# An attention scan and two feed-forward blocks on one core: another order for the first units, and levels in pairs

## The reference, cut to what matters

```
# q, k, v, f_logit: (4, 8, 768, 48), float32
f = sigmoid(f_logit)
for t in range(768):
    state = f[t][:, None] * state + outer(k[t], v[t])     # per batch and head, 48 x 48
    y[t] = q[t] @ state
x = y as (3072, 384)
h = x @ w_in                                              # 384 -> 2048
g = h if h >= 1, 0 if h <= -1, else (h + 1)**2 / 4
x = g @ w_out                                             # 2048 -> 384
out = (silu(x @ w_gate) * (x @ w_val)) @ w2_out           # 384 -> 1536 -> 384
```

## Time and profile before

| | |
|---|---|
| time, median of 3 runs | 1065.81 us (1065.61 to 1066.0) |
| the profiled execution's own time | 1066.25 us |
| its span, first to last instruction | 1064.0 us |
| TensorE busy | 1001.3 us, 94% |
| VectorE, ScalarE, GpSimd busy | 509.1, 457.1, 450.7 us |
| unit 0's scan alone | 0 to 75.08 us |
| stage 0 with unit 1's scan | 75.08 to 175.97 us |
| one later stage with a scan | 94.4 us |
| stage 5 and the second block | 553.80 to 1064.0 us |
| sizes of the opening loads (page, part 6) | gates, queries, keys 512 KB a group; q_tok, k_tok 384; eye 64; mask 80 |

### The profile page before, as it was taken

How to read it: one execution, slowest core, us unless ns; L and a number is a source line. 1 busy time by engine, 2 the same in 40 slices (tenths; PEclk the granted TensorE clock), 3 DMA queues, 4 the chain that set the end, 5 groups by cost and what they waited for, 6 DMA issues and landing times.

```text
span 1064.0 us, 19376 instructions
## 1 busy us (share of the span) xinstructions
PE 1001.3 (94%) x8008; PEld 818.2 (77%) x8008; DVE 509.1 (48%) x625; ACT 457.1 (43%) x832; POOL 450.7 (42%) x368
## 2 busy tenths in 40 slices
PE   2467899999999999999999999999999999999997
PEld 2455687778777777877888888888888888888886
DVE  7946955863793596478427522222222222222221
ACT  3459548556654855575436522122122222222221
POOL 4957963763665376356328312112112122122121
PEclk9979999999999999999999999999999999999999
DMA  9423005005101400410044010010010000000000
GB/s 359 161 88 132 1 14 207 31 2 178 72 2 38 182 31 2 131 59 2 15 165 149 30 60 1 1 60 1 1 60 1 26 34 1 30 1 1 30 1 30
DMA packets 17366, 63.50 MB, mean 60 GB/s; under 512 B 1920, under 2 KB 2176, under 8 KB 16512
## 3 DMA queue, kind: packets, MB, share of 16 engines
q1 hardware_dynamic: 17280, 62.28, 16.1%
HBM read 52.84 MB, written 9.44 MB: 59 GB/s over the span
## 4 chain that ended last, share of the span: by engine, by line
PE 82%; POOL 6%; issue 5%; ACT 3%; DVE 2%; DMA 1%; SPq 0%; POOLq 0%; ACTq 0%; DVEq 0%
PE acc L487 10%; PE acc L489 10%; PE acc L488 10%; PE bank L514 7%; PE bank L515 7%; PE bank L513 7%; PE hid L473 5%; PE hid L475 5%; PE hid L474 5%; PE bank L360 5%; PE hid L514 2%; PE hid L515 2%; PE hid L513 2%; POOL g_lo L989 2%; POOL keys L950 2%
## 5 line engine op out<-in xcount | busy, mean ns | idle before, releaser
L996 POOL TENSOR_TENSOR g_lo<-prod,g_hi 128x512 fp32r<-128x512 f32 x72 | 93.0, 1292 | 347.5 <-ACT g_hi L710 347.5
L989 POOL TENSOR_TENSOR g_lo<-act_tmp,g_hi 128x512 fp32r<-128x512 f32 x96 | 137.3, 1431 | 178.0 <-ACT g_hi L671 178.0
L892 DVE TENSOR_TENSOR sig<-sig,bank 128x512 f32<-128x512 f32 x72 | 49.5, 687 | 275.4 <-ACT sig L704 275.4
L710 ACT CAST g_hi<-prod 128x512 fp32r<-128x512 f32 x72 | 44.7, 621 | 247.8 <-PE acc L489 247.8
L950 POOL TENSOR_TENSOR keys<-keys,gates 128x512 f32<-128x512 f32 x82 | 110.4, 1347 | 47.5 <-PE bank L360 30.7
L810 DVE COPY_PREDICATED scores<-mask,bank 64x512 f32<-64x512 int32 x120 | 116.4, 970 | 20.3 <-PE bank L360 19.0
L671 ACT CAST g_hi<-act_tmp 128x512 fp32r<-128x512 f32 x96 | 59.5, 619 | 152.6 <-DVE act_tmp L880 152.6
L487 PE MATMUL acc<-g_hi,wout_hi 128*128 128x512 f32 x288 | 117.3, 407 | 7.4 <-POOL g_lo L989 7.4
L473 PE MATMUL hid<-x_hi,win_hi 128*128 128x512 f32 x288 | 118.4, 411 | 5.9 <-DVE act_tmp L880 5.9
L475 PE MATMUL hid<-x_hi,win_lo 128*128 128x512 f32 x288 | 113.2, 393 | 0.0
L474 PE MATMUL hid<-x_lo,win_hi 128*128 128x512 f32 x288 | 113.1, 393 | 0.0
(11 more groups left out here) (83 smaller groups left out, 1862.7 us busy)
## 6 DMA issues: line engine op xcount, KB each, us to landing
gates<-in_f_dram SPq DMA_DIRECT2D x12, 512.0 KB, 5.3
queries<-in_q_dram SPq DMA_DIRECT2D x12, 512.0 KB, 4.6
keys<-in_k_dram SPq DMA_DIRECT2D x12, 512.0 KB, 5.2
values<-in_v_tok_dram SPq DMA_DIRECT2D x6, 1024.0 KB, 8.5
q_tok<-in_q_tok_dram SPq DMA_DIRECT2D x12, 384.0 KB, 9.1
k_tok<-in_k_tok_dram SPq DMA_DIRECT2D x12, 384.0 KB, 9.6
x_dram<-x_out SPq DMA_DIRECT2D x6, 768.0 KB, 3.2
x_raw<-x_dram SPq DMA_DIRECT2D x6, 768.0 KB, 5.5
```

The lines of the kernel that those rows point to most:

```text
L989: pool.tensor_tensor(g_lo[:, c % RING, :], act_tmp[:, 2 + c % 2, :], g_hi[:, c % RING, :].bitcast(F32), ALU.subtract).then_inc(g_lo_done, 1)
```

## The change

1. **Opening loads.** For each group, gates, queries and keys now come before q_tok and k_tok; the identity and the mask come after all five of group 0.
2. **Unit 0's plan** is written out. The gates come first, then the copies of the first level; diagonals are summed and placed between the first levels; each `take_level` comes one step later behind the next scaling; GpSimd splits no weights during the levels; `key_values` and what follows lie in stage 0, behind its first `hidden`.
3. **Counting.** `q_gated` is a semaphore of its own, and unit 0 no longer does its last two scalings of queries, so its `outputs` do not wait for them. `keys_tok` of unit 0 has a place of its own.
4. **Unit 1.** Its plan has pairs from half slot 4; its diagonals are placed by VectorE, no longer by ScalarE; its gates are loaded before its keys, and both loads of gates and queries wait for earlier points.
5. **Weights' low parts.** GpSimd's pieces 0 to 3 of w_in come after unit 0's levels and 4 to 7 in chunks 0 to 3 of stage 0; the 8 pieces of w_out go to VectorE, in chunks 1 to 8. `state_apart` is cleared by GpSimd.
6. **Pairs.** In units 1 to 5 the two steps of a level are in one half slot on TensorE and for `scale_q`; copies, takes and `scale_k` keep one half slot each. All four `outputs` are in one half slot. `last` and the diagonals move by a slot.

```diff
@@ plans
-H_FIRST = -9
+H_FIRST = -13
+BY_VECTOR = 2
-USUAL = usual((1, 3, 5, 7, 8, 9, 10, 12, 13, 14), 16, 18, 21)
-SECOND = usual((6, 8, 9, 10, 11, 12, 13, 14, 16, 17), 19, 21, 23, place=(0, 2, 3, 4), sigmoid=(3, 4), gated=(4, 5))
-FIRST = USUAL._replace(diag=(-3, -2), sigmoid=(-3, -2), gated=(-3, -2))
+FIRST = Plan(own=(-6, -3), diag=(-4, 1), place=(-2, 2), sigmoid=(-6, -5), gated=(-6, -3),
+             copy=(-6, -4, -2, 0, 2, 4, 6, 8, 10, 12, 14, 14), step=(-4, -2, 0, 2, 4, 6, 8, 10, 12, 14),
+             take=(0, 2, 4, 6, 8, 10, 12, 14, 16, 18), scale=(-5, -1, 1, 3, 5, 7, 9, 11, 13, 15, 17, 17),
...
+SECOND = usual((4, 7, 10, 13, 15), 18, 21, 23, own=(-11, -10), diag=(-10, -9), place=(-8, 1), sigmoid=(-7, -6),
+               gated=(-6, -5))
+USUAL = usual((2, 5, 8, 11, 13), 16, 19, 21)
@@ usual: was place=(-6, -5, -4, -3), copy = step-1, take = step+1, y=(y, y, y+1, y+1)
+    two = [h for h in levels for _ in range(2)]
+    p = Plan(own=(-13, -12), diag=(-12, -11), place=(-7, -6, -5, -4), sigmoid=(-2, -1), gated=(-1, 0),
+             copy=[h + g - 2 for h in levels for g in range(2)] + [whole - 1] * 2, step=two,
+             take=[h + g + 1 for h in levels for g in range(2)], scale=two + [whole] * 2 + [last] * 2,
+             turn=[h + g for h in levels + (whole, last) for g in range(2)], whole=whole, whole_take=whole + 1,
+             last=last, last_take=last + 1, decay=y + 1, y=(y, y, y, y), y_out=(y, y, y + 1, y + 1),
@@ SyncE
         for g in range(2):
-            load_tok(0, (g,))
             load_f(0, (g,))
-            if g == 0:
-                sp.dma_start(eye[:, :], ident).then_inc(const_in, 16)
             load_q(0, (g,))
             load_k(0, (g,))
+            load_tok(0, (g,))
             if g == 0:
+                sp.dma_start(eye[:, :], ident).then_inc(const_in, 16)
                 sp.dma_start(mask[:, :], masks).then_inc(mask_in, 16)
@@ TensorE, outputs
                 pe.wait_ge(v_in, 16 * (a + 1))
-                pe.wait_ge(q_scaled, (a + 1) * SCALED_A_UNIT)
                 if a > 0:
+                    pe.wait_ge(q_scaled, scaled(a, SCALES))
@@ VectorE
-        dve.memset(state_apart[:, :, :].rearrange("p x d -> p (x d)"), 0.0).then_inc(cleared, 1)
...
+                if m == 0 and 1 <= c < 1 + W2N:
+                    split_w2(c - 1)
@@ GpSimd
+        pool.memset(state_apart[:, :, :].rearrange("p x d -> p (x d)"), 0.0).then_inc(cleared, 1)
...
-            if h >= 4 and h % 2 == 0 and h // 2 - 2 < W1N:
-                split_w1(h // 2 - 2)
+            if h == 19:
+                split_w1(0)
+            elif 23 <= h < 26:
+                split_w1(h - 22)
...
-                if m == 0 and c < W2N:
-                    split_w2(c)
+                if m == 0 and c + 4 < W1N:
+                    split_w1(c + 4)
```

More of the change, by code:

```diff
@@ L49 @@
 DVE_A_UNIT, ACT_A_UNIT = STEPS + 2, 3 + B
-SCALED_A_UNIT = 2 + SCALES
 HS = 32
-H_FIRST = -9
+H_FIRST = -13
+BY_VECTOR = 2
 Plan = namedtuple("Plan", "own diag place sigmoid gated copy step take scale turn whole whole_take last last_take "
                           "decay y y_out tk tk_out kv state state_place")
[L62 to L69, removed]
+FIRST = Plan(own=(-6, -3), diag=(-4, 1), place=(-2, 2), sigmoid=(-6, -5), gated=(-6, -3),
+             copy=(-6, -4, -2, 0, 2, 4, 6, 8, 10, 12, 14, 14), step=(-4, -2, 0, 2, 4, 6, 8, 10, 12, 14),
+             take=(0, 2, 4, 6, 8, 10, 12, 14, 16, 18), scale=(-5, -1, 1, 3, 5, 7, 9, 11, 13, 15, 17, 17),
+             turn=(-4, -2, 0, 2, 4, 6, 8, 10, 12, 14, 16, 16, 18, 18), whole=16, whole_take=17, last=18, last_take=19,
+             decay=20, y=(20, 20, 20, 20), y_out=(20, 20, 21, 21), tk=(22, 22, 22, 22), tk_out=(22, 22, 23, 23),
+             kv=HS, state=HS + 1, state_place=HS + 2)
@@ new lines, in usual @@
+def usual(levels, whole, last, y, **others):
+    two = [h for h in levels for _ in range(2)]
[4 more added lines that the diff above has]
+             last=last, last_take=last + 1, decay=y + 1, y=(y, y, y, y), y_out=(y, y, y + 1, y + 1),
+             tk=(y + 2, y + 2, y + 3, y + 3), tk_out=(y + 3, y + 3, y + 4, y + 4), kv=y + 4, state=y + 5, state_place=y + 6)
@@ L88, in turns @@
 def turns(m, h):
-    if m < 0:
-        return [(0, h)] + [(1, p) for p in range(H_FIRST, 0) if h == p + HS - 8]
-    now = []
+    now = [(0, h + HS)] if m == 0 else []
     if m + 1 < UNITS:
@@ L102, in fill, with scaled @@
     return a * FILLS + i
+def scaled(a, n):
+    return sum(SCALES if b else COPIES for b in range(a)) + n
 def merges(a, s):
@@ L426, in turn_keys @@
             pe.wait_ge(k_scaled, a * SCALES + SCALES - 1 + b // 2)
+            if a == 0 and b == 0:
+                pe.wait_ge(const_in, 16)
             for p in range(PAIRS):
@@ L438, in key_values @@
                     d = e * (P - D)
-                    last = pe.matmul(of(a, i)[rows(e), x * D:(x + 1) * D], keys_tok[:, bp, e, :],
+                    last = pe.matmul(of(a, i)[rows(e), x * D:(x + 1) * D], keys_tok[min(a, 1)][:, bp, e, :],
                                      values[:, bp, d:d + D], start=True, stop=True)
@@ L626, in attention @@
         def attention(a, h):
-            for b in range(B):
-                if a > 0 and PLANS[a].place[b] == h:
+            if a >= BY_VECTOR:
+                for b in placed(PLANS[a].place, h):
                     place_diag(a, b)
-            for g in range(2):
-                if PLANS[a].sigmoid[g] == h:
-                    sigmoid(a, g)
+            for g in placed(PLANS[a].sigmoid, h):
+                sigmoid(a, g)
             if h == PLANS[a].whole_take:
@@ L763, in gated @@
             t = group(queries, g)
-            dve.tensor_tensor(t, t, group(gates, g), ALU.mult).then_inc(q_scaled, 1)
+            dve.tensor_tensor(t, t, group(gates, g), ALU.mult).then_inc(q_gated, 1)
         def sum_own(a, g):
@@ L959, in attention @@
         def attention(a, h):
-            for g in range(2):
-                if PLANS[a].own[g] == h:
-                    own(a, g)
+            for g in placed(PLANS[a].own, h):
+                own(a, g)
             for s in placed(PLANS[a].turn, h):
```

62 lines of the change are left out of this document (35 added, 27 removed).

## The result

| | before | changed |
|---|---|---|
| median of 4 runs, us | 1065.9 | 1049.57 (1048.31 to 1050.42) |
| ratio, 95% interval | | 0.9842 [0.9825, 0.9859] |
| profiled execution, us (span) | 1066.25 (1064.0) | 1048.31 (1046.4) |
| first `hidden` | 75.08 | 69.17 |
| hidden chunk 10 of stage 0 | 138.70 | 136.02 |

The single steps were worse than the total: the start (units 0 and 1) gave 3.05 us of the span instead of 6.8, the later stages 14.55 instead of 4.7 (175.97 + 888.03 = 1064.0 before; 172.92 + 873.48 = 1046.4 now). One miss of 3.8 and one of 9.9 of opposite sign made the total look better than its parts; that is luck.

The account below looks back on a forecast made before the run. Gains were seen in unit 0's latency, TensorE's idle time in unit 1 (VectorE taken as full) and later stages, mostly TensorE's own work. Chunk 10 -6.6, outputs -0.2, later stages -4.7: -11.5, so 1054.3 us, range 1045 to 1061.

Parts of the forecast that it names:

- the 1.15 taken: Unit 0, VectorE: each scaling falls from 1.57 to 1.15 us with GpSimd's pieces gone, 12 x 0.42 = -5.0.
- 2.29: Unit 0, VectorE: group 0's placing, new in the unbroken run, costs 2.29 us, with its sum +3.2.
- `hidden` waits for VectorE about once a chunk: Unit 1: `hidden` waits about once a chunk, as the chunk's `activate` stands behind scalings and takes on VectorE.
- I see no step at which it would wait long: Unit 1: VectorE's 65.2 us follow the split of y at 66.9 without long waits; chunk 10 at 132.1, -6.6.
- rival A: VectorE eats unit 1's gain: scalings stay 1.57, pieces cost 1.66, chunk 10 at 137.3, total 1059.5; chance 0.20.
- the 137 named as the sign of a wrong forecast: Unit 1: chunk 10 coming after 137 us would show the forecast wrong, pointing to rivals A or D.
- the cost per level: Later stages: reading in which the 0.20 belongs to each level, not the change of shape, so pairs gain 0.
- Net +0.5: Stage boundaries: earlier diagonals turn the wait of 0.36 into about 1.4 and remove 0.56; +2.0 over four boundaries.
- Rival C: Later stages: a pair of halves saves nothing, +4.8 against the forecast, 1059.1; chance 0.06.
- B: Rival: TensorE bounds unit 1, VectorE keeps up and the 9.9 idle goes; -19.9, 1045.9; chance 0.14.
- D: Rival, slower: pieces at 1.66 on VectorE also lengthen GpSimd's keys; chunk 10 7.7 later, 1068.6; chance 0.05.
- E: Rival: the identity's delay and the new order cancel all over; no change, 1065.8; chance 0.03.

Follow-up runs that it names:

- E6: Changed kernel with seven of GpSimd's eight low parts of w_in made one per chunk in stage 0's first seven chunks; 1048.6 us, ratio 0.9831.
- second execution: The changed kernel run and profiled once more, with no edit; 1049.64 us, ratio 0.9833.
- E1: Changed kernel with the two halves of a masked level in units 2 to 5 in two half slots on TensorE again; 1057.9 us, ratio 0.9906.
- E4: Changed kernel with the unmasked last level of units 2 to 5 in half slot 18 instead of 19; 1053.68 us, ratio 0.9870.
- E3: Changed kernel with ScalarE placing the four diagonals of units 2 to 5 one half slot later again; 1053.73 us, ratio 0.9867.

## Why the prediction came out as it did

**Unit 0: right within 1.3 us, with two errors that cancel.** The sigmoid came at 9.86 (forecast 9.8), the last scaling ended at 53.5 (53.2), `whole` ended at 54.0 (52.7), `last_level` started at 56.7 (55.7), `outputs` at 61.4 (60.2) behind ScalarE's copies, `hidden` at 69.2 (67.9). Scalings cost 0.96 instead of the 1.15 taken: 12 x 0.19 = 2.3 less. Two placings cost 3.58 instead of 2.29: 2.6 more. The 1.3 is there by `whole`: it was to end 0.5 ahead of the last scaling and ended 0.5 behind it. The step that failed is "2.29" for an operation that ran alone before and now runs beside GpSimd.

**Unit 1: VectorE full as forecast, but not alone, and the gain too large.** VectorE was 97% busy, pieces of w_out cost 1.23 (1.2). The split of y ended at 68.3 (66.9): 1.4 late. The contents came to about what was forecast, but by other terms: the first placing and the first gating 3.2 more (E6), the scalings 1.7 less than before. "`hidden` waits for VectorE about once a chunk" did not come: there are two waits, 9.6 us in all, and behind 104.20 TensorE is busy 31.18 of 31.82. "I see no step at which it would wait long" left out the gaps, 2.1 us of idle VectorE in that stretch, 0.9 of them at its end, where chunk 10 stands behind TensorE's own `project` (133.84 to 136.02) and no longer behind an activation (over at 134.5). Chunk 10 came at 136.0, in the second execution at 138.1, not 132.1. That is near rival A's 137.3, and the second is past the 137 named as the sign of a wrong forecast. A had the number and not the terms: it kept unit 0's scalings at 1.57 and took pieces at 1.66 (measured 0.96 and 1.23). Its total was wrong because it shared the forecast's small gain of the later stages.

**Later stages: three terms too small, one with the wrong sign.** Per stage 94.44 - 90.66 = 3.78. The runs break it up: halves in pairs 1.84 (E1; forecast 5 x 0.20 = 1.0), `last` 0.94 (E4; 0.62), diagonals 0.62 (E3; -0.5). Together 3.40; 0.38 is left for the outputs in one run (0.20), which by the edges is 0.22 and by the run's length 6.25 instead of 2 x 3.19, 0.13. That last term was worked out and not tried by itself. Stage 4 gains 3.25: pairs 1.84, diagonals 0.94, `last` only 0.08. For the pairs, the cost of an edge was right (0.22 for 0.20), and what failed was to take the small products themselves as equal: one run of 64 is 0.14 shorter than two of 32. E1 refutes the cost per level. The Trainium skill (TensorEngine Tiling (Array Packing), Key Properties) says that a change of the tiling mode drains TensorE; by it a pair pays once, and the trace agrees. At the boundary the failed step is "Net +0.5": it counted ScalarE's queue ahead of one high part and made one wait of 1.4 of it, which came as 0.80, and it left out the 0.50 us that TensorE is busy longer beside two waits (E3). Why the wait is 0.80 and not 1.4 was not tried.

Rival C (a pair saves nothing) falls with E1. B had TensorE's 9.9 idle us in unit 1 go; 10.2 are there (66.85 - 56.60), though they lie ahead of 104.20, and TensorE bounds the rest. D and E fall with the result.

## What to carry to other kernels

A duration taken from a place where a neighbour engine is idle is a lower bound: price an operation that is moved by what GpSimd does at the new place. On a TensorE that has no idle time, runs of small products between large ones are worth joining: each join gave 0.37 us here (1.84 for five). Where one engine sets the pace in a stretch, look for work in it that has a later due time; moving three low parts behind the stretch gave about 2.5 us, while shifting the neighbour's work inside it gave little. Busy shares over a whole stretch hide a change of the bound inside it: cut the stretch at the last wait of TensorE before naming the engine that sets the pace.
